# Two mixture-of-experts layers behind an attention: layer two's output is turned and scaled one step later, through layer one's PSUM bank

## The reference, cut to what matters

```python
def reference(...):
    h = mab(I, x)                  # 2 x 11456 points pooled into 32 inducing points (setup phase)
    x = mab(x, h)                  # attention of every point on them
    x = moe(x, emb, tau, w1, w2)       # layer one: the one expert of largest logit
    return moe2(x, modality, w_gate, modality_bias, w1b, w2b)   # layer two: the same, other gate

# both layers, for the rows whose expert is e:
#   out[rows] = gate_w[rows] * (relu(x[rows] @ w1[e]) @ w2[e])     128 -> 1024 -> 128, 8 experts
```

## Time and profile before

| | |
|---|---|
| median of 3 runs | 1101.46 us (1101.04 to 1102.66) |
| the profiled execution | 1104.6 us, span 1102.8 us |
| mean granted TensorE clock | 0.954 |
| PE busy | 987.3 us, 90% of the span |
| DVE busy | 760.5 us, 69% |
| ACT busy | 666.7 us, 60% |
| POOL busy | 248.8 us, 23% |
| 42 loop steps | from 224.0 to 1024.6 us of the span |

### The profile page before, as it was taken

One profiled execution on the slowest core, in us unless ns is written; L12 is line 12 of the kernel. 1 busy time (PEld: TensorE's weight loads), 2 busy tenths in 40 slices (PEclk: granted clock), 3 DMA queues, 4 the chain that ended last, 5 costly groups with the idle time before them and its releaser, 6 DMA issues.

```text
span 1102.8 us, 27898 instructions
## 1 busy us (share of the span) xinstructions
PE 987.3 (90%) x6367; PEld 498.8 (45%) x6367; DVE 760.5 (69%) x2224; ACT 666.7 (60%) x1614; POOL 248.8 (23%) x461
## 2 busy tenths in 40 slices
PE   5566473789999999999999999999999999999887
PEld 4445231345444444444444444444454444444433
DVE  3545575657778687777777787777777777877654
ACT  3434163456666666766666666666666666667553
POOL 2759911211111111111111111111111111111100
PEclk9868786789999999999999999999999999999999
DMA  9999372101111101010111111010101111010000
GB/s 194 301 282 297 124 244 67 31 21 28 38 33 28 42 23 47 23 47 24 40 30 37 34 26 44 23 47 23 44 26 38 32 30 41 23 47 23 16 23 21
DMA packets 75163, 70.71 MB, mean 64 GB/s; under 512 B 33370, under 2 KB 61570, under 8 KB 75118
## 3 DMA queue, kind: packets, MB, share of 16 engines
q1 hardware_dynamic: 75118, 70.14, 23.8%
HBM read 40.55 MB, written 23.55 MB: 58 GB/s over the span
## 4 chain that ended last, share of the span: by engine, by line
PE 81%; DMA 8%; POOL 4%; issue 2%; DVE 2%; ACT 1%; SPq 1%; ACTq 0%; DVEq 0%; POOLq 0%
PE y L1273 43%; PE up L1296 22%; PE up L1286 7%; DMA GW<-in_x 3%; DMA wraw<-in_moe_w 2%; PE y L1350 2%; POOL wraw L472 2%; PE TB L1312 1%; DMA x_turned<-GW 1%; POOL W1B L476 1%; PE TB L1336 1%; PE SM L1324 1%; PE up L1212 1%; PE SM L1344 1%; DMA ind<-in_inducing 1%
## 5 line engine op out<-in xcount | busy, mean ns | idle before, releaser
L856 DVE SCALAR_TENSOR_TENSOR hlo<-up,hhi 128x500 f16<-128x500 f32 x736 | 494.0, 672 | 171.5 <-ACT hhi L594 168.7
L594 ACT ACTIVATE hhi<-up 128x500 f16<-128x500 f32 x736 | 424.5, 583 | 170.6 <-PE up L1296 84.6
L1296 PE MATMUL up<-ytb,W1B 128*128 (+1 forms) x1104 | 276.4, 381 | 11.9 <-issue 11.3
L1273 PE MATMUL y<-hhi,W2A 128*128 128x500 f16 x736 | 218.5, 379 | 10.4 <-DVE hlo L856 5.5
L1273 PE MATMUL y<-hhi,GW 128*128 128x500 f16 x736 | 215.4, 374 | 0.4 <-DVE hlo L856 0.4
L1296 PEld LDWEIGHTS up<-ytb,W1B 128*128 x1104 | 108.7, 99 | 149.0 <-issue 40.3
L1286 PE MATMUL up<-E4T,GW 128*128 (+1 forms) x368 | 139.4, 382 | 0.0
L1273 PE MATMUL y<-hlo,W2A 128*128 128x500 f16 x368 | 138.7, 377 | 0.0
L1273 PE MATMUL y<-hlo,GW 128*128 128x500 f16 x368 | 137.5, 374 | 0.0
L1273 PEld LDWEIGHTS y<-hhi,W2A 128*128 x736 | 68.2, 98 | 92.9 <-issue 46.2
L514 POOL TENSOR_TENSOR st<-ss,root 125x4 f32<-125x4 f32 x46 | 46.9, 1019 | 236.4 <-ACT TB L620 236.4
(11 more groups left out here) (165 smaller groups left out, 1066.0 us busy)
## 6 DMA issues: line engine op xcount, KB each, us to landing
wraw<-in_moe_w SPq DMA_DIRECT2D x24, 512.0 KB, 4.7
xth<-x_turned SPq DMA_DIRECT2D x46, 250.0 KB, 2.6
out<-yout SPq DMA_DIRECT2D x46, 250.0 KB
x_turned<-GW SPq DMA_DIRECT2D x10, 1000.0 KB, 13.4
GW<-in_x SPq DMA_DIRECT2D x10, 960.0 KB
W1B<-in_moe_w SPq DMA_DIRECT2D x8, 512.0 KB, 11.9
x_turned<-GW SPq DMA_DIRECT2D x2, 750.0 KB, 9.7
GW<-in_x SPq DMA_DIRECT2D x2, 720.0 KB
```

What stands on the lines that cost most here:

```text
L594: nc.scalar.activation(hhi[:, (u % UP) * CT:(u % UP + 1) * CT], ups[u % UP][:, 0:CT], ACT.Relu).then_inc(s["hi_done"], 1)
L856: nc.vector.scalar_tensor_tensor(hlo[:, o:o + CT], ups[u % UP][:, 0:CT], 0.0, hhi[:, o:o + CT], ALU.max, ALU.subtract).then_inc(s["lo_done ...
L1273: ins = mm(y[:, 0:CT], W[:, bass.ds(woff + (fb * 2 * C + o), C)], h[:, k * CT:(k + 1) * CT], start=opens and fb == 0 and n == 0, stop=fb = ...
L1296: ins = mm(ups[k][:, 0:CT], W1B[:, bass.ds(woff + (wl * F + fb * P), P)], ytb[:, bass.ds(yoff + yl * CW, CT)], start=n == 0, stop=n == 2)
```

## The change

Transposes and result of chunk c move into step c+1. TensorE transposes `yT` behind unit 3 into `y1` (free there, since layer one's result of the step before was read at the step's head), ScalarE does result halves of two copies behind units 6 and 7, from `y1`. Layer one's first product, down(8), opens `y1` anew and therefore waits for `result_ready`; layer two's first product, down(0), waits only for `result_copied` (`yT` written). There is a step 46 that holds only the last transposes and result. Step 0, which has no result before it, is no longer in the loop but written out.

```diff
-            for c in range(-4, 0):
+            for c in range(-4, 1):
                 step(c)
-            with eng.Fori(0, NCH - 4) as c:
+            with eng.Fori(1, NCH - 4) as c:
...
             def store(z):
-                sp.wait_ge(s["result_ready"], z + 2)
+                sp.wait_ge(s["result_ready"], z + 3)
...
-                def result():
-                    act.wait_ge(s["gate_steps"], CG * (c + 3))
-                    act.wait_ge(s["out_free"], c + 1)
-                    act.wait_ge(s["result_transposed"], c + 1)
-                    for j in range(TJ):
-                        ins = nc.scalar.activation(yout[:, j * C:(j + 1) * C], y2[0:TQ, j * C:(j + 1) * C], ACT.Copy,
-                                                   scale=coef[:, bass.ds(parity(c) * TJ + j, 1)])
-                    ins.then_inc(s["result_ready"], 1)
+                def result(j0):
+                    if j0 == 0:
+                        act.wait_ge(s["gate_steps"], CG * (c + 2))
+                        act.wait_ge(s["out_free"], c)
+                        act.wait_ge(s["result_transposed"], c)
+                    for j in (j0, j0 + 1):
+                        ins = nc.scalar.activation(yout[:, j * C:(j + 1) * C], y1[0:TQ, j * C:(j + 1) * C], ACT.Copy,
+                                                   scale=coef[:, bass.ds(parity(c + 1) * TJ + j, 1)])
+                    if j0:
+                        ins.then_inc(s["result_ready"], 1)
...
+                            6: [lambda: result(0)] if last else [], 7: [lambda: result(2)] if last else [],
                             8: [lexps] if rx or ry else [], 10: [lambda: yt(after())] if l2 else [],
-                            11: [exps] if xq else [], 15: [result] if l2 else []}
+                            11: [exps] if xq else []}
...
+                    def before():
+                        pe.wait_ge(s["result_ready"], c + 2)
+                    return up, down_of(W2A, woff, y1, opens, before if opens and (not isinstance(c, int) or c >= 1) else None)
...
                     def before():
-                        pe.wait_ge(s["result_ready"], c + 1)
+                        pe.wait_ge(s["result_copied"], c + 1)
...
-                        ins = nc.tensor.transpose(y2[0:TQ, j * C:(j + 1) * C], yT[:, j * TQ:(j + 1) * TQ],
+                        ins = nc.tensor.transpose(y1[0:TQ, j * C:(j + 1) * C], yT[:, j * TQ:(j + 1) * TQ],
...
-                         5: when(xq, scores), 8: when(joint, counts), 12: when(l2, out_transposes)}
+                         3: when(not isinstance(c, int) or c >= 1, out_transposes),
+                         5: when(xq, scores), 8: when(joint, counts)}
...
             all_steps(pe, pe_step)
+            pe_step(NCH)
```

More of the change, by code:

```diff
@@ L636, in exps @@
                         s["chunk_exp"], 1)
-                def result():
-                    act.wait_ge(s["gate_steps"], CG * (c + 3))
-                    act.wait_ge(s["out_free"], c + 1)
-                    act.wait_ge(s["result_transposed"], c + 1)
-                    for j in range(TJ):
-                        ins = nc.scalar.activation(yout[:, j * C:(j + 1) * C], y2[0:TQ, j * C:(j + 1) * C], ACT.Copy,
-                                                   scale=coef[:, bass.ds(parity(c) * TJ + j, 1)])
-                    ins.then_inc(s["result_ready"], 1)
+                def result(j0):
[8 more added lines that the diff above has]
+                        ins.then_inc(s["result_ready"], 1)
                 def tasks(after):
+                    last = not isinstance(c, int) or c >= 1
                     return {4: [squares] if rx else [],
+                            6: [lambda: result(0)] if last else [], 7: [lambda: result(2)] if last else [],
                             8: [lexps] if rx or ry else [], 10: [lambda: yt(after())] if l2 else [],
-                            11: [exps] if xq else [], 15: [result] if l2 else []}
+                            11: [exps] if xq else []}
                 def step(mixed):
@@ L688, in act_step @@
                     step(False)
-            act.sem_inc(s["result_ready"], 1)
+            act.sem_inc(s["result_ready"], 2)
+            act.sem_inc(s["result_copied"], 1)
             all_steps(act, act_step)
+            act_step(NCH)
         @block.vector
@@ L1287, in up @@
                                   e4, start=True, stop=True)
-                    return up, down_of(W2A, woff, y1, opens)
+                    def before():
+                        pe.wait_ge(s["result_ready"], c + 2)
+                    return up, down_of(W2A, woff, y1, opens, before if opens and (not isinstance(c, int) or c >= 1) else None)
                 def layer2(woff, opens):
```

## The result

The changed kernel takes **1129.8 us** in the median (1127.9 to 1135.6, 4 runs); the kernel before, on the same chip, 1101.65. The ratio is 1.0269, with a 95% interval of 1.0238 to 1.0299. It is slower, as forecast, but by 28.2 us where 14.2 were forecast, and outside the range of 1107 to 1122. The profiled execution took 1129.2 us, with a span of 1127.0 against 1102.8.

What follows compares the result with a forecast made beforehand. TensorE, busy 99.34 of 100 us in the loop, was taken as the bound; loop steps +6.7, step 0 written out +5.1 and tail +2.4 sum to +14.2, so 1101.46 becomes 1115.7 us, range 1107 to 1122.

Steps and rivals of the forecast that it cites:

- step 0 written out: Entries into step 0 and the loop's first pass: two stalling entries instead of one, +5.1 us.
- nor do the one-layer steps: Branches over the mixed half: entries stall where a long half is jumped first time; other loop passes and one-layer steps don't.
- A loop step, +0.15: Loop step: gap before down(8) filled, transposes' 0.44 replaced by a 0.39 gap before down(14); +0.15 us per step.
- Only 0.07 of slack is left: the transposes cover a wait: End of a loop step: transposes after down(13) cover down(14)'s wait for lo(15), with 0.07 us of slack.
- The tail, +2.4: Steps 44, 45 and the last result: later hi(7) and the wait for store 44 cost +2.4 us, between +0.5 and +3.
- Saves its transposes and the wait ahead of them at its end: Step 44: loses like step 45 but saves transposes and their wait at its end; +0.4 us taken.
- Faster: Rival: the gap at down(8) is filled and no new one opens, -0.29 us per step; 1096.5 us, chance 0.07.
- ScalarE becomes the bound: Rival, units 7 to 11: lo(7) to lo(10) come later, 0.4 us at down(8) per step; 1132 us, chance 0.08.
- The loop stalls at every pass: Rival: the loop's code grows and each pass stalls, 41 x 3.4 us and more; over 1240 us, chance 0.02.
- No stall for step 0: Rival: written-out step 0 follows on without a loop's border and adds no stall; 1110.6 us, chance 0.08.
- the change cancels: Rival: down(14)'s 0.15 us delay less a smaller gap elsewhere, 0 to -0.17 per step; 1101 to 1109 us, chance 0.07.

Runs made afterwards that it cites:

- move alone: Changed kernel with step 0 back in the loop (loop from 0), its first pass turning a cleared `yT`: 1115.0 us, ratio 1.0118 to the kernel before.
- the shifted kernels: Semaphore increments as filler at the head of TensorE's program: 64 in the changed kernel, 1120.1 us; 96 in the kernel before, 1109.47 us.
- changed kernel shifted by 64: Changed kernel with 64 semaphore increments that nobody waits for at the head of TensorE's program: 1120.1 us, ratio 1.0168 to the kernel before.
- own waits: Each of a step's last two downs waits for its own lo instead of both for lo(15): changed kernel 1112.45 us, kernel before 1091.9 us.
- ups first: Kernel before with up(u+4) ahead of down(u) instead of behind it, eight slots for `hhi` and `hlo`: 1091.43 us, ratio 0.9909.

## Why the prediction was right in direction and wrong in size

**The step that failed is "step 0 written out": "After the change two such entries stand where one stood ... +5.1".** For the two entries themselves it was near: steps 0 and 1 together lost 5.9, though by a stall and a second fetch. What was missing is that the written-out step shifts all code behind it. I had taken from three stalls the rule that the mixed half must be long, and that "nor do the one-layer steps" stall; those had only been lucky in their place. The two more stalls at steps 44 and 45, with the slow clock behind them, cost 9.0: from step 43 to the end of the span are 64.6 us, against 55.6 in the kernel with the move alone. The entries into 42 and 43 gave 3.0 back: their branches took 3.3 and 3.4 us instead of 4.0 and 4.4, and behind the first the ups ran in 2.70 instead of 4.39. No run shows that the change did that, and it may be chance. The experiment that only writes step 0 out shows +15.0 where the term had +5.1; the shifted kernels show that the place of the code does it. Against the sum of 14.2 the profiles show 0.8 more for steps 0 and 1, 1.0 more in the loop, 2.4 more from step 43 on even without new stalls (see the tail), 9.0 for the new stalls, 3.0 less at 42 and 43 and 0.1 less ahead of step 0: 24.3, the difference of the spans to 0.1.

**A loop step, +0.15: right in mechanism, 0.19 measured.** down(8) was put at 12.37 after the step's start and came at 12.34; the gap before down(14) was put at 0.39 and is 0.38; hi(7) was put 1.2 later and is 1.14 later; ScalarE's idle time was put at 1.4 and is 1.29. The small step that failed is the one that holds the border at 0.38 in both kernels: down(14) came 0.09 after its old place, not 0.15, and the border grew from 0.38 to 0.47. Counted along the chain, up(15) came 0.15 later (15.79 after the step's start instead of 15.64), and from there to the next step's first up took 3.39 instead of 3.35: 0.15 + 0.04. For steps 1 to 42 the term was 6.3; 7.3 are measured in 39 of them.

**"Only 0.07 of slack is left: the transposes cover a wait"** is confirmed by the kernel without transposes. It didn't go far enough: at the border there was no slack at all.

**The tail, +2.4.** In step 45 the mechanism is right. down(6) has a gap of 0.97 instead of 0.38, and the last result waits for SyncE's wait for store 44. Rows of the kernel after, beside the earlier trace rows:

```profile
1117.59 5.46 SPq L354 DMA_DIRECT2D out<-yout  x2
...
1121.61 1.14 ACT L644 ACTIVATE yout<-y,coef 125x128 f32<-125x128 f32 x4 [1.66 <-SPq L357]
```

From the step's first up to that result are 16.88 us, against 12.17 before. Of the 4.7, 2.5 are the twelve ups in 5.18 instead of 2.70 us, at the lower clock; the rest is about the 2.0 that the term had for it. Step 44 was put at +0.4, and the kernel with the move alone shows +1.1. "Saves its transposes and the wait ahead of them at its end" failed: the flags of the next step bind there. In that kernel the counts start at 1088.97, the last of the flags at 1089.82 and the next ups at 1091.39, 2.42 after the counts; before it is 2.38, under cover of which the transposes had cost nothing:

```profile
1088.97 0.25 PE L1355 MATMUL SM<-oneh,ones 125*1 125x16 f16 x4
...
1089.82 0.14 DVE L1049 TENSOR_TENSOR flags<-fsum,fmax 1x2 int32<-1x2 f32 x1
1091.39 0.39 PE L1307 MATMUL up<-ytb,W1B 128*128 128x500 f16 x1 [2.17 <-issue]
```

**The slow ups of step 45 don't need the stall.** Their whole group, in the kernel with the move alone and in the changed kernel shifted by 64:

```profile
1091.39 4.38 PE L1307 MATMUL up<-ytb,W1B 128*128 128x500 f16 x12 [2.17 <-issue]
...
1093.17 5.18 PE L1307 MATMUL up<-ytb,W1B 128*128 128x500 f16 x12 [2.13 <-issue]
```

The branches ahead of them took only 0.42 and 0.43 us. What stands ahead is TensorE's idle time of 2.2 us at the end of step 44; before, it was 0.50 and 0.93, with the transposes between. The prediction put the clock behind the end of step 44 at nothing. In the kernel with the move alone it is 1.7 of the 2.4 us that the steps from 43 on lost beyond their terms; most of the rest is step 44. It doesn't come each time: without transposes TensorE idled 2.14 us there, and the ups ran in 2.70.

**The rivals.** "Faster" was wrong for this kernel, but its mechanism is real: without the chain at the border the move is worth 0.19 per step. "ScalarE becomes the bound" gives 1132, near the measured 1129.8, and is nonetheless wrong: down(8) came no later than worked out. "The loop stalls at every pass" is refuted: 39 passes of 19.18. "No stall for step 0" is refuted by the two long entries into steps 0 and 1, and "the change cancels" by the period, which grew by 0.19.

## What to carry to other kernels

When an edit writes code out or makes it longer, don't stop at its own branch: look at the duration of every branch behind it, and compare with a kernel that is shifted by filler alone, since the place of the code was worth up to 10 us here. Before a piece of work is moved off a stretch, measure the stretch from the last operation that feeds other engines to the first that follows the wait; if this distance is the same with and without the work, it is a chain, and neither moving nor deleting the work gains anything until the chain is cut (own waits, or its head issued earlier). A border that looks normal because it is the same in every step may be a wait in every step.

## What the runs showed of the hardware

- A branch that had to fetch code took 3.3 to 4.6 us in these runs, against 0.208 in the median, and twelve ups behind it took up to 5.18 us instead of 2.70. In the stretch from 1104 to 1114 of the kernel after, behind 5.20 us in which TensorE was idle, the granted clock was 0.67 of the full 2.4 GHz, so part of it ran at 1.2 GHz. The lower clock didn't follow every stall: in the kernel with only step 0 written out, TensorE idled 2.79 us ahead of step 44, and the ups took 2.70.

```profile
1104.00:1114.00 10.00, 9.27 (x31) 3.75 (x32) 4.36 (x10) 3.52 (x6) 0.00 (x0) 0.67 0.01 2
```

- The price of a fetch varies at one place of the code: the branch into the loop's first pass took 3.71 us in the kernel before, 3.90 with the move alone, 4.50 with ups first and 4.64 without transposes, and none of these edits moves it. In the last two another packet of the queue had started 0.3 and 0.2 us after the branch, ahead of the one that was needed, which took 2.1 us; where no other was in flight it took 0.9 to 1.6. The kernel before had medians near 1101.4 in every job, but single runs from 1096.6 to 1106.9; whether that comes from the fetches was not tested.
- The loop's jump back and its jump over the mixed half never stalled after the first pass, in any kernel. Its body of 3.8 blocks was not fetched again: the kernel after has no packet of the queue between 265.0 and 1038.2, the kernel before none between 233.9 and 1025.0. A first entry of the same length does need a fetch. How much code stays at hand was not tested.
- TensorE's sequencer runs ahead of the products, but a semaphore wait holds it back, and with it a branch that stands behind the wait: in the changed kernel with own waits down(14) and down(15) run without a gap, and still the next up comes 0.57 us after the last product, with no wait of its own that the profile names ("issue").
